# Attention before two expert layers: key-feature sums moved to GpSimd, key exponents read from the projection bank, one maximum for q and k

## The chip, the cores and the metric

The kernel runs on one core of one Trainium2 chip. The metric is the device time of the whole program in microseconds; the times shown are medians over several runs. The profiled execution is a run of its own, with its own time.

## The reference, cut to what matters

```python
def phi(x):                                   # q, k: (4, 8, 576, 64); w_phi: (64, 128)
    proj = np.einsum('bhsd,df->bhsf', x, w_phi)
    proj = proj - np.max(np.abs(proj), axis=-1, keepdims=True)
    return np.concatenate([np.exp(proj), np.exp(-proj)], axis=-1)
q_p, k_p = phi(q), phi(k)
kv = np.einsum('bhsf,bhsd->bhfd', k_p, v)
z = np.sum(k_p, axis=2)
num = np.einsum('bhsf,bhfd->bhsd', q_p, kv)
den = np.einsum('bhsf,bhf->bhs', q_p, z)[..., None] + 1e-06
attn = num / den                              # -> x, (2304, 512)
```

After it come a dense layer (512 to 2048 to 512 with a relu6 gate) and a routed layer with 8 experts. Neither is touched.

## The kernel before, in words

**Tiling.** The 32 heads go in 16 pairs (u = 0 to 15). Each pair has 9 tiles of 128 rows: four for each head, and a tail tile with the last 64 rows of both heads. A tile's 128 features are doubled by the two signs s of the exponent. The tiles are worked in three groups, `GROUPS = [(8, 1), (0, 4), (4, 4)]`: group 0 is the tail tile, groups 1 and 2 have four tiles each (the first two tiles of each head, then the last two).

**One pair, by engine.** TensorE projects a group of q and k into two PSUM banks, one for each, with no second copy (`projections`, L593). VectorE (`differences`, L1080) takes the largest absolute value of each row of k, subtracts it into `dif` in SBUF, and does the same for q. ScalarE makes the key features `pk` from `dif` (`k_features`, L904, two instructions a group). TensorE transposes the q differences (`dif_transposes`, L612) and ScalarE turns these into query features `pq` (`q_features`, L894). TensorE sums keys times values over the tiles (`kv_sums`, L624, bank KVB) and the key features alone (`z_sums`, L639, bank ZB, products with ones, each tile in its own strip of 32 rows). ScalarE copies both to SBUF (`copy_kvt`, L914). TensorE transposes the first (`kv_transposes`, L653) and multiplies the second by `z_pick`, which adds the strips and spreads them over 64 columns (`z_transposes`, L658). ScalarE copies the result (`copy_kv`, L920). TensorE forms numerators and denominators together (`numerators`, L667, `numerator_tails`, L677), and VectorE divides (`pair_out`, L1118) into `x_sb`.

**Order.** Every engine has a program written out by hand. Steps of pair u+1 are put between those of pair u; each engine works strictly in its order, and only semaphores join them. TensorE's order is `both` at L685, ScalarE's L951, VectorE's L1169. `pair_loop` (L310) runs pairs 0 and 1, a loop over pairs 2 to 7, `middle`, and pairs 8 to 14 with `phase` set; the last pair has a program of its own. GpSimd makes constants at the start; in this stage it then only takes two maxima over the partitions (L497, L499).

**Beside it.** The weights of the dense layer arrive in pieces of 128x1024 (SyncE, `load_pieces`). In pairs 0 to 7 VectorE searches each piece for its maximum (`piece_max_of`, L1129). Then come the maximum over the partitions and five small steps for the scale (`weight_scales`, L1160). In pairs 8 to 15 ScalarE writes the high part of each piece (`piece_hi_of`, L926) and VectorE the low part (`piece_lo_of`, L1136). VectorE also keeps the maximum of v (`v_max`, L1121), whose scale is made in pair 14 (`x_scales`, L1199). In the last pair x is scaled (`x_hi` L933, `x_lo` L1208) and transposed (`x_transpose`, L576) for the dense layer.

Of the kernel before, what the change touches and what calls it, by code (L numbers as in the profile page):

```python
# [34 lines left out]
MT = 4  # L35
# [31 lines left out]
def moe_program(nc, qkt_in, v, w_phi, w_in, w_out, w_gate, w_ogate, w1, w2, out, rows, split):  # L67
# [8 lines left out]
    with ctx:  # L76
# [29 lines left out]
        kvt_sb = part(2 * 2 * F).rearrange("p (z s f) -> p z s f", z=2, s=2)  # L106
        kv_sb = part(4 * 2 * DH).rearrange("p (s z h d) -> p s z h d", s=2, z=2, h=2)
        den = part(2 * PT).rearrange("p (a t) -> p a t", a=2)
        mx = part(2 * PT).rearrange("p (w t) -> p w t", w=2)
        v_sb = part(2 * (PT + 1) * DH).rearrange("p (a t d) -> p a t d", a=2, t=PT + 1)  # L110
        tail_ones = part(2 * 32).rearrange("p (h c) -> p h c", h=2)
        z_pick = part(P)
        dif = part(2 * 2 * PT * F).rearrange("p (a w t f) -> p a w t f", a=2, w=2, t=PT)
        assert used[0] <= 3 * UW
        qkt = part(2 * PT * P).rearrange("p (a n) -> p a n", a=2)
# [93 lines left out]
        max_ready = sem("max_ready")  # L209
        dif_transposed = sem("dif_transposed")  # L210
# [3 lines left out]
        z_summed = sem("z_summed")  # L214
# [73 lines left out]
        PROJ, TB, KVB, ZB, NB = (0, 1), (2, 3), 4, 5, 6  # L288
# [160 lines left out]
        def _(pool):  # L449
# [5 lines left out]
            last_row, last_token = pool.alloc_register("last_row"), pool.alloc_register("last_token")  # L455
            pool.reg_mov(last_row, DUMMY - 1)
            pool.reg_mov(last_token, N - 1)
# [14 lines left out]
            step(nc.gpsimd.memset(tail_ones[:], 0.0))  # L472
            step(nc.gpsimd.memset(tail_ones[0:DH, 0, :], 1.0))
            step(nc.gpsimd.memset(tail_ones[DH:P, 1, :], 1.0))
            step(nc.gpsimd.memset(z_pick[:], 0.0))
            for j in range(4):
                step(nc.gpsimd.memset(z_pick[32 * j:32 * j + 1, DH * (j // 2):DH * (j // 2) + DH], 1.0))
# [18 lines left out]
            pool.wait_ge(max_in, 1)  # L496
            nc.gpsimd.partition_all_reduce(s_max[:, 0:3], s_red[:, 0:3], P, RMAX).then_inc(max_out, 1)  # L497
            pool.wait_ge(max_in, 2)
            nc.gpsimd.partition_all_reduce(s_max[:, 3:4], s_red[:, 3:4], P, RMAX).then_inc(max_out, 1)  # L499
# [72 lines left out]
        def _(pe):  # L572
# [20 lines left out]
            def projections(u, a, g):  # L593
# [6 lines left out]
                if g > 0:  # L600
                    pe.wait_ge(dif_ready, u * 6 + 2 * g)
                elif not isinstance(u, int) or u > 0:
                    pe.wait_ge(dif_ready, u * 6)
# [8 lines left out]
            def dif_transposes(u, a, g):  # L612

                t0, n = GROUPS[g]
                pe.wait_ge(dif_ready, u * 6 + (2 * g + 2))
# [4 lines left out]
                for t in range(n):  # L620
                    last = nc.tensor.transpose(ps[:, TB[g % 2], t * P:(t + 1) * P], dif[:, a, 0, t0 + t, :], ident[:])
# [16 lines left out]

            def z_sums(u):  # L639

                if not isinstance(u, int) or u > 0:
                    pe.wait_ge(tails_ready, u)
                for t in (0, 1, MT):
                    for hh in range(2):
                        for j in range(2 if t < MT else 1):
                            lhs = ones[:, 0:32] if t < MT else tail_ones[:, hh, :]
                            row = DH * hh + 32 * j
                            last = nc.tensor.matmul(ps[row:row + 32, ZB, 0:2 * F], lhs,  # L648
                                                    pk[:, at(hh, t + 2 * j), :, :].rearrange("p s f -> p (s f)"),
                                                    start=t == 0, stop=t == (MT, 1)[j])  # L650
                last.then_inc(z_summed, 1)

            def kv_transposes(u):  # L653
                pe.wait_ge(kvt_ready, u * 2 + 1)
                for s in range(2):
                    nc.tensor.transpose(ps[:, KVB, 2 * s * P:2 * s * P + P], kvt_sb[:, 0, s, :], ident[:])
# [844 lines left out]
```

## Time and profile before

| | |
|---|---|
| median of 3 runs | 963.38 us (962.7 to 967.49) |
| profiled execution, its own time | 964.04 us |
| its span | 962.5 us, 20311 instructions |
| TensorE products | 869.5 us busy (90%) |
| TensorE weight loads | 574.2 us (60%) |
| VectorE | 580.6 us (60%) |
| ScalarE | 388.8 us (40%) |
| GpSimd | 74.9 us (8%), 120 instructions |
| mean granted TensorE clock | 0.959 |

The span runs from the first to the last instruction; the execution's time is slightly longer. Busy shares are averages over all stages: the attention stage is the first quarter. A group of instructions carries the line of the code that issues it, the tiles it writes and reads ("arena" holds all tiles of this stage but the raw inputs to it), their shapes, and the count. A product in f32 shows as two records. The idle time in brackets is that of the engine just before the row, with what ended it.

### The profile page before, as it was taken

The numbers are of one execution on the slowest core, as the hardware profiler recorded it, in microseconds if no ns is written. First come the engines' busy times: TensorE is split into PE (matmuls) and PEld (weight loads), VectorE is DVE, ScalarE is ACT, GpSimd is POOL, SyncE is SP. The second block draws the span as 40 slices with busy tenths as digits, with TensorE's granted clock in tenths as the row PEclk, the third lists the DMA queues.
The fourth block names the chain that finished last, engine by engine and source line by source line (L and its number), as shares of the span: only waits on it lengthen the run. The fifth ranks groups of instructions, "written<-read, shape, count | busy, mean of one in ns | idle before, by whom it ended". The sixth has DMA issues, their size and how long they took to land.

```text
span 962.5 us, 20311 instructions
## 1 busy us (share of the span) xinstructions
PE 869.5 (90%) x7480; PEld 574.2 (60%) x7481; DVE 580.6 (60%) x1202; ACT 388.8 (40%) x666; POOL 74.9 (8%) x120
## 2 busy tenths in 40 slices
PE   5999999998899999997999999992499999999990
PEld 3777777777455555553555555552377777777770
DVE  3778788875795987985987987545131322222223
ACT  2445456656456565664656665522010100011011
POOL 1000000000000001001001001011011111111111
PEclk9999999999999999998999999995599999999995
DMA  6243344331565366465266452554317342664110
GB/s 191 92 161 113 132 160 161 128 123 36 192 235 202 143 234 223 162 230 216 97 226 224 156 206 121 201 182 150 103 46 299 137 162 98 228 251 176 44 34 13
DMA packets 44062, 151.36 MB, mean 157 GB/s; under 512 B 7710, under 2 KB 12062, under 8 KB 37856
## 3 DMA queue, kind: packets, MB, share of 16 engines
q1 hardware_dynamic: 38320, 134.14, 39.2%
q0 software_dynamic: 5520, 16.31, 4.9%
q8 instruction: 41, 0.67, 0.3%
q14 instruction: 21, 0.17, 0.1%
q10 hardware_dynamic: 160, 0.07, 0.0%
HBM read 104.72 MB, written 47.21 MB: 158 GB/s over the span
## 4 chain that ended last, share of the span: by engine, by line
PE 57%; PEld 14%; DVE 10%; issue 8%; DMA 4%; PEldq 3%; ACT 2%; SPq 1%; DVEq 0%; POOL 0%; POOLq 0%; ACTq 0%
PE ps L743 19%; PE ps L732 17%; PEld ps L834 10%; PE ps L607 4%; PE ps L634 4%; PE ps L673 3%; PEld ps L846 3%; DVE arena L1087 3%; PE ps L834 2%; PE ps L648 2%; DVE arena L1094 2%; PE ps L846 2%; DMA arena<-split 1%; DVE u_mx L1253 1%; PE ps L661 1%
## 5 line engine op out<-in xcount | busy, mean ns | idle before, releaser
L732 PE MATMUL ps<-arena,w_in_sb 128*128 128x384 f16 x1152 | 203.5, 329 | 6.0 <-issue 6.0
L743 PE MATMUL ps<-w_out_sb,arena 128*128 128x512 f16 x576 | 172.3, 381 | 9.1 <-DVE stage L1341 9.1
L732 PEld LDWEIGHTS ps<-arena,w_in_sb 128*128 128x128 f16 x1152 | 111.4, 99 | 81.7 <-issue 9.2
L1067 ACT ACTIVATE w_in_sb<-ps 128x512 f16<-128x512 f32 x50 | 29.5, 597 | 257.0 <-PE ps L834 241.3
L834 PEld LDWEIGHTS ps<-w_in_sb,arena 128*128 128x128 f16 x2112 | 124.0, 100 | 9.8 <-issue 5.0
L834 PE MATMUL ps<-w_in_sb,arena 128*128 128x128 f16 x2112 | 125.9, 223 | 4.3 <-DMA arena<-split 2.4
L846 PE MATMUL ps<-arena,w_in_sb 128*128 128x512 f16 x528 | 117.5, 379 | 0.0
L743 PE MATMUL ps<-w_out_sb,stage 128*128 128x512 f16 x288 | 109.7, 381 | 0.0
L1442 DVE SCALAR_TENSOR_TENSOR w_in_sb<-ps,w_in_sb 128x512 f16<-128x512 f32 x50 | 34.3, 691 | 113.7 <-ACT w_in_sb L1067 113.7
L743 PEld LDWEIGHTS ps<-w_out_sb,arena 128*128 128x128 f16 x576 | 55.9, 98 | 68.9 <-issue 11.7
L1033 ACT ACTIVATE arena<-relu 128x384 f16<-128x384 f32 x96 | 50.2, 523 | 106.6 <-DVE relu L1336 106.6
L1336 DVE SCALAR_TENSOR_TENSOR relu<-relu,ps 128x384 f32<-128x384 f32 x96 | 53.0, 552 | 64.8 <-ACT relu L1027 64.2
L846 PEld LDWEIGHTS ps<-arena,w_in_sb 128*128 128x128 f16 x528 | 50.8, 98 | 57.1
L1027 ACT ACTIVATE relu<-ps,three,s_h 128x384 f32<-128x384 f32 x96 | 63.8, 665 | 51.2 <-PE ps L732 48.8
L1280 DVE SCALAR_TENSOR_TENSOR arena<-arena,u_up 128x1024 f16<-128x1024 f32 x64 | 79.2, 1278 | 0.0
L1253 DVE TENSOR_REDUCE u_mx<-arena 128x1 f32<-128x1024 f32 x64 | 74.8, 1211 | 3.9 <-DMA arena<-in_moe_w 3.9
L1087 DVE TENSOR_REDUCE arena<-ps 128x4 f32<-128x512 f32 (+1 forms) x96 | 52.9, 551 | 39.2 <-PE ps L607 39.1
L1018 ACT ACTIVATE arena<-arena,u_up 128x1024 f16<-128x1024 f32 x64 | 69.8, 1137 | 2.9 <-DVE u_up L1272 2.4
L673 PE MATMUL ps<-arena 128*128 128x128 f32 x512 | 66.4, 284 | 3.6 <-ACT arena L924 3.6
L1452 DVE TENSOR_SCALAR w_in_sb<-ps,stage 128x512 f32<-128x512 f32 x25 | 18.7, 750 | 78.5 <-PE ps L846 78.5
L673 PEld LDWEIGHTS ps<-arena 128*128 128x128 f32 x512 | 60.4, 194 | 9.2 <-ACT arena L924 7.3
L911 ACT ACTIVATE arena<-arena 128x512 f32<-128x512 f32 (+1 forms) x96 | 45.1, 522 | 45.3 <-DVE arena L1094 45.3
(175 smaller groups left out, 927.5 us busy)
## 6 DMA issues: line engine op xcount, KB each, us to landing
arena<-in_moe_w SPq DMA_DIRECT2D x16, 2048.0 KB, 13.1
split<-arena SPq DMA_DIRECT2D x16, 2048.0 KB, 7.4
arena<-split SPq DMA_DIRECT2D x32, 1024.0 KB, 5.8
arena<-in_qkt SPq DMA_DIRECT2D x15, 576.0 KB, 6.2
stage<-in_moe_w_in SPq DMA_DIRECT2D x16, 512.0 KB, 4.3
stage<-in_moe_w_out SPq DMA_DIRECT2D x16, 512.0 KB, 5.4
w_in_sb<-rows POOLq DMA_DIRECT2D x25, 257.0 KB, 3.0
arena<-in_v SPq DMA_DIRECT2D x32, 128.0 KB, 4.5
```

The source lines that it names most:

```text
L673: last = nc.tensor.matmul(ps[:, NB + hh, t * 2 * DH:(t + 1) * 2 * DH], pq[:, s, c:c + P], kv_of(s, hh), start=s == 0, stop=s == 1)
L732: last = nc.tensor.matmul(ps[:, HB[f % GB], 0:BN], w_in_sb[:, lw, c, f * P:(f + 1) * P], xt[:, a, c, lx, :], start=c == 0 and lw + lx == 0 ...
L743: last = nc.tensor.matmul(ps[:, YB + r, :], g_sb[lg_][:, f % GB, r * P:(r + 1) * P], w_out_sb[:, lw, f, :], start=f == 0 and lg_ + lw == 0 ...
L834: last = nc.tensor.matmul(ps[:, 2 + 2 * a + f // 4, f % 4 * P:(f % 4 + 1) * P], w1_sb[b][:, lw, c, f * P:(f + 1) * P], xgt[:, a, lx, c, :] ...
L846: last = nc.tensor.matmul(ps[:, 6 + a, :], hg[:, a, lh, f, :], w2_sb[b][:, lw, f, :], start=f == 0 and lh + lw == 0, stop=f == EFC - 1 and ...
L1018: nc.scalar.activation(split_sb[:, 0, q_ * Q:(q_ + 1) * Q], raw[b][:, q_ * Q:(q_ + 1) * Q], ACT.Copy, scale=u_up[:, b:b + 1]).then_inc(u_h ...
L1027: nc.scalar.activation(relu3[:, f % GB, :], ps[:, HB[f % GB], 0:BN], ACT.Relu, bias=three[:, 0:1], scale=s_h[:, 0:1]).then_inc(relu3_ready, 1)
L1033: nc.scalar.mul(g_sb[0][:, f % GB, :], relu3[:, f % GB, :], CG / 6.0).then_inc(g_hi, 1)
L1087: nc.vector.tensor_reduce(mx[:, w, t0:t0 + n], src, AX.X, ALU.max, apply_absolute_value=True).then_inc(max_ready, 1)
L1253: nc.vector.tensor_reduce(u_mx[:, q_:q_ + 1], raw[b][:, q_ * Q:(q_ + 1) * Q], AX.X, ALU.max, apply_absolute_value=True).then_inc(u_searche ...
L1280: nc.vector.scalar_tensor_tensor(out=split_sb[:, 1, cols], in0=raw[b][:, cols], scalar=u_up[:, b:b + 1], in1=split_sb[:, 0, cols], op0=ALU ...
L1336: nc.vector.scalar_tensor_tensor(out=relu3[:, f % GB, :], in0=relu3[:, f % GB, :], scalar=6.0, in1=ps[:, HB[f % GB], 0:BN], op0=ALU.min, o ...
```

## The change

The key features are made straight from the projection bank in PSUM: for each tile and sign one exponent over 128x128, with the row maximum as bias (negated by a small new VectorE instruction into `k_neg` for the plain sign). The key half of `dif` and its subtraction are gone. One maximum is taken over the q and k banks together. The sums of the key features over the tiles are additions on GpSimd into `pk_sum` (SBUF), and TensorE multiplies these by 64 columns of ones straight into the place of the spread sums; `z_sums` of before, its copy, `tail_ones`, `z_pick` and `z_transposes` are gone. The high parts of the weight pieces are written by GpSimd, not ScalarE. The two maxima over the partitions stand in GpSimd's new program between its additions. TensorE's order in a pair changes: the key-value sums now come before the projections of group 0, and the transposes of group 2 before the key-value transposes. The projections also wait for `pk_ready`.

```diff
@@ gpsimd
+            def sums(u, n, out, x, y):
+                nc.gpsimd.tensor_tensor(out, x, y, ALU.add).then_inc(sum_step, 1)
+                pool.wait_ge(sum_step, u * 4 + n)
+            def sums_first(u):
+                pool.wait_ge(pk_ready, u * 3 + 2)
+                if not isinstance(u, int) or u > 0:
+                    pool.wait_ge(kv_transposed, u)
+                sums(u, 1, pk_sum[:], pk[:, 0:4:2], pk[:, 1:4:2])
+                for hh in range(2):
+                    rows_ = slice(DH * hh, DH * hh + TAIL)
+                    sums(u, 2 + hh, pk_sum[rows_, hh], pk_sum[rows_, hh], pk[rows_, 2 * MT])
+            def sums_second(u):
+                pool.wait_ge(pk_ready, u * 3 + 3)
+                sums(u, 4, pk_sum[:], pk_sum[:], pk[:, 4:8:2])
+                nc.gpsimd.tensor_tensor(pk_sum[:], pk_sum[:], pk[:, 5:8:2], ALU.add).then_inc(pk_summed, 1)
+            def piece_hi_of(u, a):
+                pool.wait_ge(w_scale, 1)
+                pool.wait_ge(stage_loaded[a], (u - a) * 16 + 32)
+                for w, dst in ((0, w_in_flat), (1, w_out_flat)):
+                    nc.gpsimd.tensor_scalar(dst[:, 0, bass.ds((u - PAIRS // 2) * Q, Q)], stage[:, a, w, :], s_up[:, w:w + 1], None,
+                                            ALU.mult).then_inc(piece_hi, 1)
+            def both(u, a, phase):
+                sums_second(u)
+                if isinstance(u, int) and u == PAIRS - 2:
+                    pool.wait_ge(max_in, 2)
+                    nc.gpsimd.partition_all_reduce(s_max[:, 3:4], s_red[:, 3:4], P, RMAX).then_inc(max_out, 1)
+                if phase:
+                    piece_hi_of(u, a)
+                sums_first(u + 1)
...
+            sums_first(0)
+            both(0, 0, 0)
+            both(1, 1, 0)
+            with pool.Fori(1, PAIRS // 4) as i:
+                both(i * 2, 0, 0)
+                both(i * 2 + 1, 1, 0)
+            weights_max()
+            for u in range(PAIRS // 2, PAIRS - 1):
+                both(u, u % 2, 1)
+            last_pair()
@@ tensor, projections
-                    pe.wait_ge(dif_ready, u * 6 + 2 * g)
+                    pe.wait_ge(dif_ready, u * 3 + g)
+                    pe.wait_ge(pk_ready, u * 3 + g)
@@ tensor, new z_sums
             def z_sums(u):
+                pe.wait_ge(pk_summed, u + 1)
+                for s in range(2):
                     for hh in range(2):
+                        c = (2 * s + 1) * P + DH * hh
+                        last = nc.tensor.matmul(ps[:, KVB, c:c + DH], pk_sum[:, hh, s, :], ones[:, 0:DH], start=True, stop=True)
@@ tensor, both
                 dif_transposes(u, a, 1)
+                kv_sums(u, a)
                 if more:
                     projections(u + 1, 1 - a, 0)
-                kv_sums(u, a)
-                z_sums(u)
+                dif_transposes(u, a, 2)
                 kv_transposes(u)
+                z_sums(u)
                 if more:
                     projections(u + 1, 1 - a, 1)
                 else:
...
-                z_transposes(u)
-                dif_transposes(u, a, 2)
@@ scalar, k_features
-                act.wait_ge(dif_ready, u * 6 + (2 * g + 1))
+                act.wait_ge(neg_ready, u * 3 + (g + 1))
                 if g == 0 and (not isinstance(u, int) or u > 0):
                     act.wait_ge(kv_summed, u)
-                    act.wait_ge(z_summed, u)
-                for s in range(2):
-                    last = nc.scalar.activation(pk[:, t0:t0 + n, s, :], dif[:, a, 1, t0:t0 + n, :], ACT.Exp, scale=1.0 - 2.0 * s)
+                    act.wait_ge(pk_summed, u)
+                for t in range(n):
+                    for s in range(2):
+                        bias = (k_neg, mx[:, 1])[s]
+                        last = nc.scalar.activation(pk[:, t0 + t, s, :], ps[:, PROJ[1], t * F:(t + 1) * F], ACT.Exp,
+                                                    bias=bias[:, t0 + t:t0 + t + 1], scale=1.0 - 2.0 * s)
@@ vector, differences
+                dve.wait_ge(projected, u * 6 + (2 * g + 2))
+                src = ps[:, PROJ[0]:PROJ[0] + 2, 0:n * F].rearrange("p w (t f) -> p w t f", t=n)
+                nc.vector.tensor_reduce(mx[:, :, t0:t0 + n], src, AX.X, ALU.max, apply_absolute_value=True).then_inc(max_ready, 1)
+                dve.wait_ge(max_ready, u * 3 + (g + 1))
+                nc.vector.tensor_scalar(k_neg[:, t0:t0 + n], mx[:, 1, t0:t0 + n], -1.0, None, ALU.mult).then_inc(neg_ready, 1)
...
+                nc.vector.tensor_tensor(dif[:, a, t0:t0 + n, :], src[:, 0],
+                                        mx[:, 0, t0:t0 + n, None].to_broadcast([P, n, F]), ALU.subtract).then_inc(dif_ready, 1)
```

## Rows read from the trace of the kernel before

**Rows 1.** Busy time by stretch: PE, PEld, DVE, ACT, POOL; clock; DMA.

```profile
60.00:100.00 40.00, 38.42 (x389) 29.59 (x390) 31.91 (x66) 17.95 (x45) 0.00 (x0) 1.00 0.44 145
```

**Rows 2.** Timeline of TensorE over one pair: start, duration, instruction.

```profile
87.39 0.49 PE L607 MATMUL ps<-wphi_sb,arena 64*128 64x128 f32 x4 [0.30 <-DVE arena L1094]
...
90.12 1.07 PE L648 MATMUL ps<-arena,ones 128*32 128x256 f32 x16
...
91.55 0.44 PE L656 MATMUL ps<-ident,arena 128*128 128x128 f32 x2
91.92 1.16 PE L607 MATMUL ps<-wphi_sb,arena 64*128 64x128 f32 x16
...
93.56 0.60 PE L621 MATMUL ps<-ident,arena 128*128 128x128 f32 x4
94.40 2.05 PE L673 MATMUL ps<-arena 128*128 128x128 f32 x16 [0.24 <-ACT arena L924]
...
96.97 1.16 PE L607 MATMUL ps<-wphi_sb,arena 64*128 64x128 f32 x16
98.06 2.05 PE L673 MATMUL ps<-arena 128*128 128x128 f32 x16
...
100.95 0.49 PE L607 MATMUL ps<-wphi_sb,arena 64*128 64x128 f32 x4 [0.30 <-DVE arena L1094]
```

**Rows 3.** Timeline of TensorE's weight loads in the routing step.

```profile
361.98 0.30 PEld L778 LDWEIGHTS ps<-onehot,ones 128*128 128x128 f32 x2
```

**Rows 4.** Timeline of VectorE in the same pair.

```profile
98.16 0.69 DVE L1087 TENSOR_REDUCE arena<-ps 128x4 f32<-128x512 f32 x1 [1.18 <-PE ps L607]
...
100.89 0.15 DVE L1103 TENSOR_SCALAR arena<-ps 128x1 f32<-128x1 f32 x1
```

**Rows 5.** Timeline of VectorE and GpSimd at the maximum of the weights.

```profile
131.21 1.21 DVE L1131 TENSOR_REDUCE w_mx<-stage 128x1024 f32 x1
...
132.99 0.39 POOL L497 PARTITION_ALL_REDUCE s_max<-s_red  x1 [125.45 <-DVE s_red L1164]
```

**Rows 6.** Groups by shape on ScalarE: count, busy us, mean ns, idle before.

```profile
L911 ACT ACTIVATE arena<-arena 128x512 f32<-128x512 f32 x64 | 36.9, 630 | 42.6 <-DVE arena L1094 42.6
L900 ACT ACTIVATE arena<-ps 128x512 f32<-128x512 f32 x64 | 34.7, 600 | 0.3 <-PE ps L621 0.3
...
L1004 ACT ACTIVATE yrow<-stage,y_up 128x512 f16<-128x512 f32 x18 | 11.6, 707 | 1.8 <-DVE y_up L1236 1.8
...
L900 ACT ACTIVATE arena<-ps 128x128 f32<-128x128 f32 x32 | 6.8, 262 | 0.0
```

**Rows 7.** Timeline of ScalarE: four query exponents in a row.

```profile
100.66 1.40 ACT L900 ACTIVATE arena<-ps 128x128 f32<-128x128 f32 x4
```

**Rows 8.** Groups by shape on GpSimd.

```profile
L528 POOL MEMSET stage<- 128x513 f32 x1 | 0.6, 555 | 0.0
...
L488 POOL CAST ident<-ident 128x128 f16<-128x128 f32 x1 | 0.3, 289 | 0.1
```

**Rows 9.** Timeline of TensorE after the maximum of the weights.

```profile
138.29 1.16 PE L607 MATMUL ps<-wphi_sb,arena 64*128 64x128 f32 x16 [0.57 <-DVE arena L1094]
```

**Rows 10.** Timeline of VectorE in pair 14, around the maximum of v.

```profile
214.41 0.81 DVE L1126 TENSOR_REDUCE v_mx<-arena 128x1 f32<-128x640 f32 x1
...
217.33 0.68 DVE L1087 TENSOR_REDUCE arena<-ps 128x4 f32<-128x512 f32 x1
```

**Rows 11.** Timeline of TensorE from the last projections to the last numerators.

```profile
220.12 1.16 PE L607 MATMUL ps<-wphi_sb,arena 64*128 64x128 f32 x16 [0.31 <-DVE arena L1094]
...
230.01 0.83 PE L590 MATMUL ps<-ident,yrow 128*128 128x128 f16 x12 [2.10 <-DVE yrow L1211]
...
232.41 2.89 PE L673 MATMUL ps<-arena 128*128 128x128 f32 x16
```

**Rows 12.** Groups by shape on VectorE: the low part of a weight piece.

```profile
L1139 DVE SCALAR_TENSOR_TENSOR w_in_sb<-stage,s_up,w_in_sb 128x1024 f32 x6 | 7.7, 1277 | 0.0
```

More of the change, by code:

```diff
@@ L105, in moe_program @@
         pq = part(2 * PT * P).rearrange("p (s n) -> p s n", s=2)
-        kvt_sb = part(2 * 2 * F).rearrange("p (z s f) -> p z s f", z=2, s=2)
+        kvt_sb = part(2 * F).rearrange("p (s f) -> p s f", s=2)
+        pk_sum = part(2 * 2 * F).rearrange("p (h s f) -> p h s f", h=2, s=2)
         kv_sb = part(4 * 2 * DH).rearrange("p (s z h d) -> p s z h d", s=2, z=2, h=2)
@@ L620, in dif_transposes @@
                 for t in range(n):
[L621 removed]
+                    last = nc.tensor.transpose(ps[:, TB[g % 2], t * P:(t + 1) * P], dif[:, a, t0 + t, :], ident[:])
                 last.then_inc(dif_transposed, 1)
@@ L637, in kv_sums, with kv_transposes @@
                 last.then_inc(kv_summed, 1)
+            def kv_transposes(u):
+                pe.wait_ge(kvt_ready, u + 1)
+                for s in range(2):
+                    nc.tensor.transpose(ps[:, KVB, 2 * s * P:2 * s * P + P], kvt_sb[:, s, :], ident[:])
             def z_sums(u):
-                if not isinstance(u, int) or u > 0:
-                    pe.wait_ge(tails_ready, u)
-                for t in (0, 1, MT):
+                pe.wait_ge(pk_summed, u + 1)
+                for s in range(2):
                     for hh in range(2):
[L645 to L654, printed above, removed]
-                for s in range(2):
-                    nc.tensor.transpose(ps[:, KVB, 2 * s * P:2 * s * P + P], kvt_sb[:, 0, s, :], ident[:])
-            def z_transposes(u):
-                pe.wait_ge(kvt_ready, u * 2 + 2)
-                for s in range(2):
-                    last = nc.tensor.matmul(ps[:, KVB, (2 * s + 1) * P:(2 * s + 2) * P], kvt_sb[:, 1, s, :], z_pick[:], start=True, stop=True)
+                        c = (2 * s + 1) * P + DH * hh
+                        last = nc.tensor.matmul(ps[:, KVB, c:c + DH], pk_sum[:, hh, s, :], ones[:, 0:DH], start=True, stop=True)
                 last.then_inc(kv_transposed, 1)
@@ L981, in last_pair @@
                     copy_xt(0, 0, c, X0[c])
-                for w in range(2):
-                    piece_hi_of(u, a, w)
                 nc.scalar.activation(wg_sb[:, 0], wg_raw[:], ACT.Copy, scale=s_up[:, 2:3]).then_inc(wg_hi, 1)
@@ L1079, in _, with differences @@
         def _(dve):
[L1080 removed]
+            def differences(u, a, g):
                 t0, n = GROUPS[g]
[L1083 to L1096 removed]
+                dve.wait_ge(projected, u * 6 + (2 * g + 2))
[3 more added lines that the diff above has]
+                nc.vector.tensor_scalar(k_neg[:, t0:t0 + n], mx[:, 1, t0:t0 + n], -1.0, None, ALU.mult).then_inc(neg_ready, 1)
+                if g == 0 and (not isinstance(u, int) or u > 1):
+                    dve.wait_ge(dif_transposed, u * 3 - 3)
+                nc.vector.tensor_tensor(dif[:, a, t0:t0 + n, :], src[:, 0],
+                                        mx[:, 0, t0:t0 + n, None].to_broadcast([P, n, F]), ALU.subtract).then_inc(dif_ready, 1)
             def normalise(u, a, b, j):
```

102 lines of the change are left out of this document (38 added, 64 removed).

## The prediction

> **What bounds the kernel now.** I read the page first (engine shares, the 40 slices), then busy time by stretch, then the timeline of one steady pair engine by engine, the waits, and the two places where GpSimd takes a maximum. The attention stage, which alone is changed, ends near 240 us. From 60 to 100 us TensorE is busy 38.42 of 40 us, VectorE 31.91, ScalarE 17.95, GpSimd not at all [rows 1]. One pair repeats every 13.56 us (87.39 to 100.95) [rows 2]. I take it apart by start times: projections of group 0 with the key-value sums 2.73, key sums (L648) 1.43, their transposes (L656) 0.37, projections of group 1 1.09, spreading transposes (L661) 0.55 (what is left before 93.56), query transposes of group 2 0.60 and a wait of 0.24, numerators and tails 2.57, projections of group 2 1.09, other numerators and transposes 2.59, a wait of 0.30 for the difference of q. The sum is 13.56. So TensorE sets the pace, with 0.54 of waiting; what it no longer has to do is a gain only until a chain through another engine sets in.
>
> **TensorE's edits.** The key sums (1.43) and spreading (0.55) go. In their place stand 4 products, 8 records of 128x128 f32 weights against 64 columns. No such shape is in the trace. A record of the numerators, same weights and 128 columns, takes 2.05/16 = 0.13, nearer 0.12 without the last one's tail; one of the projections, half the rows, 1.09/16 = 0.07 [rows 2]; two loads of such weights before 24 columns take 0.30, so at most 0.15 each [rows 3]. Loads, not columns, set it, so I take 0.11, just under the numerators: 0.88 in all (0.55 to 1.2). 1.10 us of work per pair is saved, and moving the projections of group 0 behind the sums removes the 0.30 wait. Nothing else on TensorE changes in amount.
>
> **The chain that takes over.** Projection banks are single. Until now VectorE read them and freed them; now ScalarE reads the key bank for its exponents, and TensorE waits for pk_ready before it writes the next group. I walk it from the start of a group of 4: TensorE to VectorE 1.19 (96.97 to 98.16), about 0.06 more as q is projected last [rows 2, 4]; one maximum over 1024 values 1.21, as the maximum of the same size in the weight search [rows 5]; the sign flip, a 128-row by few-column instruction, 0.15 with 0.05 ahead of it [rows 4]; a hand-over of 0.04; then 8 exponents of 128x128 where two of 128x512 stood. From PSUM one takes 0.262 alone, the 512 form 0.600 [rows 6]; four of them in a row (two of each) took 1.40 against 1.72 added, so neighbours overlap by 0.11 [rows 7]. A per-partition operand costs 0.08 (0.707 against 0.630, both from SBUF) to 0.107 (against 0.600) [rows 6]. I take 0.09: 0.25 a piece, 7 x 0.25 + 0.35 = 2.10. With 0.04 to TensorE the chain is 4.84. Bounds: 4.1 if the operand costs nothing in a row of them (7 x 0.15 + 0.26 = 1.3), 5.2 if it costs twice as much and the overlap halves.
> Between group 1 and group 2 TensorE has 1.09 + 2.57 = 3.66 to do. So it now waits 1.2 us there in each pair, which eats the saving.
>
> **The pair after.** Count from the start of group 2's projections. Group 2 1.09; numerators and transposes 2.59, to 3.68; sums of tiles 0, 1 and tail (six tenths of 2.31) to 5.07, while pk_ready of group 2 comes at 4.84, so no stall; sums and group 0 end at 6.41; transposes of group 2 7.01; the key-value transposes 7.38 (their copy on ScalarE ends by 6.7: exponents to 4.8, four of q to 6.1, and a copy of 256 columns, under 0.6). Now TensorE needs GpSimd's sum. GpSimd starts its two additions at 4.86. The first half (one addition of 512 and two of 256 on 64 rows) lies in the 4.8 us before, with room. Then products to 8.26, group 1, and 4.84 later the next group 2: 13.10. ScalarE's copy of kv (0.6) and query exponents end 1.8 after group 1 starts, before their 2.7; VectorE's search (1.21) and v maximum end at 9.4, its next work is due at 9.5. Gain: 0.46 a pair.
>
> **The additions.** GpSimd has never added here. Bounds per addition of 512: 0.56, one write of 513 columns; 2.3, two inputs each at four times the 0.289 of a 128-column cast [rows 8]. I take four casts, 1.16, since a cast already reads and writes: done at 4.86 + 2 x 1.16 + 0.1 = 7.28, against 7.38. There is just no stall. The sum's arrival also frees ScalarE, whose exponents of the next pair's group 0 now wait for it with the copy of kv queued behind them: 7.28 + 0.6 = 7.9, before group 1 at 8.26, so nobody waits for that. The Trainium skill ("GPSIMD Engine Reference", Performance versus the Vector engine) gives 4497 ns for a two-input f32 addition over 2048 columns and about 2.6 cycles an element; that is an estimate of 1.1 to 1.2 for 512, on the value taken, and no row here shows one. Above 1.21 each further 0.1 costs 0.2 a pair: a stall of 2.2 a pair at the upper bound.
> Moving the scaling of weight pieces to GpSimd frees ScalarE of work (two pieces of 1024 columns a pair, from u = 8) that was already off the path; on GpSimd they fill 7.3 to at most 12 (eight casts each, 2.3), before its next sum at 13.1. The small constants that fall away at the start were nobody's wait, and SyncE's loads follow the same semaphores in the same order, now slightly earlier: both at nothing.
>
> **Two places where GpSimd's order costs.** (a) The maximum over the weights now stands in GpSimd's stream before the second half of pair 8. VectorE hands it over only after the differences of group 0 of pair 9 and the last piece's search. The search starts at 7.35 of that pair; from there to GpSimd's reduction is 1.78 (131.21 to 132.99), the reduction 0.39 [rows 5], then two additions, 2.4: sum at 11.9 instead of 7.3. TensorE loses 4.5 once, where it lost 0.57 before [rows 9]. (b) The maximum over v in pair 14: VectorE's v maximum starts at 8.5, and from its start to the next differences 2.92 pass (214.41 to 217.33) [rows 10], so these begin at 11.4 instead of 9.5: 1.9 on the chain that now has no slack, against 0.31 before [rows 11]. Together 5.5 more than before.
> **The last pair.** The input transposes wait for the scaled x as before: 9.89 after the last projections [rows 11]. After them stood spreading and query transposes until the numerators, 232.41 - 230.01 = 2.40; now only the transposes themselves, 0.83 less the tail of the last, about 0.7 as an estimate: 1.7 less.
>
> **Sum**, against the profiled execution (span 962.5, its time 964.04, 0.66 over the median of 963.38): 15 pairs x 0.46 = 6.9 less, 1.7 less, 5.5 more: 3.1 less, 960.9, which is 960.3 against the median. Some 0.5% (4.8 us) is what can be told from no change, so faster means under 958.6, slower over 968.2.
>
> **Rivals.** *GpSimd's additions become the bound* (slower). It decides from 1.31 us an addition: each 0.1 over 1.21 costs 0.2 x 15 plus 0.2 in pair 8, so 3.2. At 1.5 the result is 960.3 + 9.3 = 969.6. For it: two inputs have to be read, and the upper bound lies far off; against it: four casts hold their fixed time four times, an addition once.
> *VectorE and GpSimd hold each other up.* From pair 9 VectorE's low part (two inputs in SBUF, 1.28 [rows 12]) and GpSimd's high part start within 0.1 us of each other, at 7.3. If one must stand still while the other runs, VectorE loses up to a high part, 1.2 to 2.3 by the cast, less its 0.1 of slack: the next maximum comes 1.5 later in pairs 9 to 13, and x's low part in the last pair by 1: 8 more, 968.5. For it: both read the same stage tile in that moment; against it: which starts first is open, and if VectorE does, nothing is lost. The Trainium skill ("SBUF — State Buffer", Who interferes with whom) states this as an exclusive lock when VectorE has two SBUF inputs and GpSimd reads SBUF; no row here shows a GpSimd read beside such an instruction, so the trace neither agrees nor differs; by the rule the time is this rival's if GpSimd starts first, and the forecast's if VectorE does.
> *The exponents are cheaper in a row* (the operand's 0.09 hides behind the one before): the chain falls to 4.1 and with half of that to 4.5; 0.4 to 0.7 a pair more, 949 to 955, say 954. For it: the 0.262 overlap nearly half; against it: 0.707 against 0.630 is plain.
> *The change brings nothing*: the kept time is lost to small stalls on VectorE, whose margins at 9.4 and 4.84 are 0.1 and 0.2: 963.5.
>
> **Chances.** Forecast 0.40, additions the bound 0.20, cheap exponents 0.20, lock 0.14, nothing 0.06. Forecast alone: 957 to 964. The range goes from 952 to 971, which leaves out the cheapest exponents and additions over 1.55. Faster: 0.20 + 0.12 of the forecast = 0.32; same: 0.27 + 0.06 + 0.07 of the two slower rivals = 0.40; slower 0.28.
>
> **What would show it.** Starts of group 2's projections 13.1 apart with a TensorE idle of 1.2 just before, released by ScalarE: the chain is right. Idle before the 4 new products: the additions are too long, and their mean says by how much. Exponents about 0.35 each, 0.25 apart. Pair 8 some 4.5 longer. VectorE idle or late before the group 1 maximum only from pair 9: the lock. Wrong if the wait before group 2 is under 0.8, or if pairs of the first and second half differ by over 0.3.

## The result and the profile after

| | before | after |
|---|---|---|
| median | 963.04 us (960.31 to 967.49) | 998.35 us (996.15 to 999.17) |
| ratio | | 1.0359, interval 1.0315 to 1.0402 |
| profiled span | 962.5 us | 996.1 us |
| TensorE products busy | 869.5 us | 860.6 us |
| ScalarE busy | 388.8 us | 401.8 us |
| GpSimd busy | 74.9 us | 209.7 us |

The changed kernel is 3.6% slower. I had forecast 960.3 us and had given slower a chance of 0.28; even my range ended at 971. Hardly any of the loss is in the steady pair. TensorE's projections of group 2 are a mark that both traces have. In pair 1 they start at 27.25 us (before 29.07), in pair 8 at 124.09 (before 124.08): what the seven pairs between lose, 1.8 us, the start had won. Nearly all of the 33.6 us of span are lost in three places, and at each of them GpSimd changes between additions and the maximum over the partitions.

GpSimd's timeline after, around the maximum of the weights (start us, us, engine, line, operation, shapes, count, and in brackets the idle time before it with what ended it):

```profile
124.03 2.86 POOL L492 TENSOR_TENSOR arena<-arena 128x512 f32<-128x512 f32 x3 [6.04 <-ACT arena L951]
133.20 0.39 POOL L528 PARTITION_ALL_REDUCE s_max<-s_red  x1 [6.31 <-DVE s_red L1186]
143.94 1.25 POOL L492 TENSOR_TENSOR arena<-arena 128x512 f32<-128x512 f32 x1 [10.35 <-issue]
145.26 1.26 POOL L507 TENSOR_TENSOR arena<-arena 128x512 f32<-128x512 f32 x1
```

The reduction takes 0.39 us, as in [rows 5]. The addition behind it has all its data, yet it starts 10.35 us later, and the idle time is put down to "issue", which means that nothing the profile shows ended it. TensorE's timeline after, in the same pair (it answers to [rows 9]):

```profile
131.11 0.38 PE L692 MATMUL ps<-ident,arena 128*128 128x128 f32 x2
146.58 1.97 PE L700 MATMUL ps<-ones,arena 128*128 128x64 f32 x8 [15.09 <-POOL arena L507]
148.48 2.08 PE L657 MATMUL ps<-wphi_sb,arena 64*128 64x128 f32 x16
150.49 2.55 PE L712 MATMUL ps<-arena 128*128 128x128 f32 x16
...
154.58 1.16 PE L657 MATMUL ps<-wphi_sb,arena 64*128 64x128 f32 x16 [0.95 <-ACT arena L951]
```

TensorE stands for 15.09 us where I had allowed 4.5. Behind the stall its records also run slow, 2.08 us for projections that take 1.16 elsewhere; in the busy times by stretch the granted clock of 140 to 180 us is 0.86, with 1.00 in the 40 us of [rows 1], and taken finer it is 0.50 from 146 to 150 us, 0.61 to 152 and 1.00 behind. By their starts these products, projections and numerators take 2.3 us more than in a steady pair. From group 2 of this pair to that of the next are 30.49 us, 16.3 more than before.

The second place is pair 14, the third the first unit of the dense layer. GpSimd's timeline after:

```profile
229.93 1.26 POOL L507 TENSOR_TENSOR arena<-arena 128x512 f32<-128x512 f32 x1
236.99 0.38 POOL L521 PARTITION_ALL_REDUCE s_max<-s_red  x1 [5.80 <-issue]
244.33 2.85 POOL L514 TENSOR_SCALAR w_in_sb<-stage,s_up 128x1024 f16<-128x1024 f32 x1 [6.96 <-issue]
...
290.87 0.38 POOL L552 PARTITION_ALL_REDUCE u_all<-u_red  x1 [26.48 <-issue]
```

TensorE's timeline after, from the last projections on (it answers to [rows 11]):

```profile
242.58 2.08 PE L657 MATMUL ps<-wphi_sb,arena 64*128 64x128 f32 x16 [6.57 <-ACT arena L951]
...
253.52 1.60 PE L684 MATMUL ps<-arena 128*64 128x256 f32 x8 [3.69 <-ACT arena L951]
...
259.00 1.48 PE L638 MATMUL ps<-ident,yrow 128*128 128x128 f16 x12
260.28 2.02 PE L712 MATMUL ps<-arena 128*128 128x128 f32 x8
```

Group 2 of the last pair is 18.99 us behind that of pair 14 (before 14.03, [rows 11]), and from there to the last numerators are 17.70 us (before 12.29). The account against before: the start 1.8 less, seven pairs 1.8 more, pair 8 16.3, pairs 9 to 13 1.2 (69.01 against 67.80), pair 14 5.0, the last pair 5.4; together 27.9 at the last numerators. The first reduction of the dense layer, at 254.98 before, comes 35.9 later, the third 34.0 later, the end 33.6.

The steady pair after, in TensorE's timeline (it answers to [rows 2]):

```profile
96.44 1.16 PE L657 MATMUL ps<-wphi_sb,arena 64*128 64x128 f32 x16 [1.28 <-ACT arena L951]
...
103.45 0.38 PE L692 MATMUL ps<-ident,arena 128*128 128x128 f32 x2
104.22 1.10 PE L700 MATMUL ps<-ones,arena 128*128 128x64 f32 x8 [0.39 <-POOL arena L507]
105.26 1.16 PE L657 MATMUL ps<-wphi_sb,arena 64*128 64x128 f32 x16
...
110.27 1.16 PE L657 MATMUL ps<-wphi_sb,arena 64*128 64x128 f32 x16 [1.28 <-ACT arena L951]
```

The period is 13.83 us, with the wait of 1.28 on ScalarE's exponents that I had forecast (1.2), and one of 0.39 on GpSimd that I had not. The other engines in this pair, in the timeline after, show how GpSimd's sum comes to be late:

```profile
98.91 0.36 DVE L1113 TENSOR_SCALAR arena<-arena 128x4 f32<-128x4 f32 x1
...
99.30 2.17 ACT L951 ACTIVATE arena<-ps,arena 128x128 f32<-128x128 f32 x8 [3.00 <-DVE arena L1113]
...
101.55 1.28 POOL L492 TENSOR_TENSOR arena<-arena 128x512 f32<-128x512 f32 x1 [2.31 <-ACT arena L951]
...
102.90 1.26 POOL L507 TENSOR_TENSOR arena<-arena 128x512 f32<-128x512 f32 x1
```

### The profile page after: what moved, and what is told of

Its sections match the earlier page's. It is cut to its first block, busy times and chain, and to the rows that moved or that the text cites. A ratio compares the mean times of both kernels' runs of the same rounds, so it can differ in the third digit from the quotient of the medians.

```text
span 996.1 us, 20022 instructions
## 1 busy us (share of the span) xinstructions
PE 860.6 (86%) x7224; PEld 575.5 (58%) x7225; DVE 561.7 (56%) x1154; ACT 401.8 (40%) x826; POOL 209.7 (21%) x208
## 4 chain that ended last, share of the span: by engine, by line
PE 44%; issue 14%; PEld 14%; DVE 8%; POOL 6%; ACT 5%; DMA 3%; PEldq 3%; SPq 1%; POOLq 0%; ACTq 0%; DVEq 0%
PE ps L781 17%; PE ps L770 15%; PEld ps L872 10%; ACT arena L951 4%; POOL arena L492 4%; PEld ps L884 3%; PE ps L657 3%; DVE arena L1111 2%; POOL arena L507 2%; PE ps L872 2%; PE ps L700 2%; PE ps L884 2%; DMA arena<-split 1%; DVE u_mx L1275 1%; DVE y_mx L1253 1%
## 5 line engine op out<-in xcount | busy, mean ns | idle before, releaser
L951 ACT ACTIVATE arena<-ps,arena 128x128 f32<-128x128 f32 x288 | 79.5, 380 | 115.6 <-DVE arena L1113 81.8
L1111 DVE TENSOR_REDUCE arena<-ps 128x8 f32<-128x1024 f32 (+1 forms) x48 | 46.0, 958 | 79.7 <-PE ps L657 79.7
L492 POOL TENSOR_TENSOR arena<-arena 128x512 f32<-128x512 f32 (+1 forms) x64 | 64.6, 1009 | 101.2 <-ACT arena L951 88.4
L657 PE MATMUL ps<-wphi_sb,arena 64*128 64x128 f32 x576 | 49.0, 306 | 34.3 <-ACT arena L951 29.8
L552 POOL PARTITION_ALL_REDUCE u_all<-u_red x16 | 7.7, 483 | 326.1 <-DVE u_red L1279 299.6
```

The lines of the kernel that those rows point to most:

```text
L492: nc.gpsimd.tensor_tensor(out, x, y, ALU.add).then_inc(sum_step, 1)
L657: done = nc.tensor.matmul(ps[:, PROJ[w], t * F:(t + 1) * F], qkt[DH * w:DH * w + DH, a, c:c + P], wphi_sb[DH * w:DH * w + DH, :], start=Tr ...
L951: last = nc.scalar.activation(pk[:, t0 + t, s, :], ps[:, PROJ[1], t * F:(t + 1) * F], ACT.Exp, bias=bias[:, t0 + t:t0 + t + 1], scale=1.0 ...
L1111: nc.vector.tensor_reduce(mx[:, :, t0:t0 + n], src, AX.X, ALU.max, apply_absolute_value=True).then_inc(max_ready, 1)
```

## The experiments

Two theories. *Theory 1*: on GpSimd a change between the additions (or the scaling) and the reduction costs 6 to 10 us each way, and this is the whole loss. *Theory 2*, on the steady pair: the sums on GpSimd are a gain, and the exponents from the projection bank give it back, since their chain ends later than TensorE's work.

**Constants in place of the reductions.**

```diff
-                nc.gpsimd.partition_all_reduce(s_max[:, 0:3], s_red[:, 0:3], P, RMAX).then_inc(max_out, 1)
+                nc.gpsimd.tensor_copy(s_max[:, 0:3], s_known[:, 0:3]).then_inc(max_out, 1)
...                                                          # and the same for 3:4
```

> The changed kernel, with its two maxima over the partitions in this stage left out: GpSimd copies constants of the right exponent in their place, at the same point of its order. Theory 1: what costs most is not the reduction (0.39) but the time around it, in which GpSimd issues nothing that the trace shows: 10.35 us after the first reduction, 5.8 before the second and 6.96 after it. A plain copy has no such time. Then TensorE's wait in pair 8 falls from 15.1 to about 4.7, VectorE's wait for the v scale from 4.2 to under 0.5, and its wait of 6.4 for the high part in pair 14 goes: some 20 to 23 us less, 976 to 979. Rival: the waits come from the order of GpSimd's program, as predicted, and from how full it is; then the copy saves only the two reductions, about 1 us, and the time stays at 997.

Measured: 979.01 us, ratio 1.0172 (1.0147 to 1.0197). GpSimd's timeline of this kernel:

```profile
133.39 0.18 POOL L532 COPY s_max<-s_known 128x3 f32<-128x3 f32 x1 [6.25 <-DVE s_red L1190]
133.54 1.26 POOL L496 TENSOR_TENSOR arena<-arena 128x512 f32<-128x512 f32 x1
```

With a copy in the place of the reduction the next addition starts at once, TensorE's stall falls from 15.09 to 4.45 us (I had forecast 4.5 for a reduction without any such gap), and 19 us are gone. So the gaps are there and cost that much; that the wait for the maximum itself made the whole stall is out. But they are not the whole loss, as theory 1 had it. TensorE's timeline of this kernel:

```profile
136.20 1.97 PE L704 MATMUL ps<-ones,arena 128*128 128x64 f32 x8 [4.45 <-POOL arena L511]
138.09 2.08 PE L661 MATMUL ps<-wphi_sb,arena 64*128 64x128 f32 x16
```

The stall is now the one that I forecast, and yet the records behind it are slow again: the granted clock is 0.50 from 136 to 142 us, and by their starts the same steps take 2.9 us more than in a steady pair. My prediction had no term for that. Of the 16.8 us left over the kernel before, 8.8 stand at group 2 of the last pair (228.92 against 220.12, 6.2 of them from pair 8), and the first unit's reduction, at 271.05 with 26.38 of "issue" ahead of it, is 16.1 late: the third place is still there.

**The reduction called once ahead of the dense layer.**

```diff
 def last_pair():
     ...
+    nc.gpsimd.partition_all_reduce(warm[:, 1:2], warm[:, 0:1], P, RMAX)   # result unused
```

> The changed kernel, with one more maximum over the partitions, of a scratch column, at the end of GpSimd's attention program. Theory 1: the first use of the reduction after ordinary instructions costs about 6 us; put where GpSimd is idle it is hidden, and the first unit maximum of the dense layer comes about 6 us earlier after its request, which gives back the 4.8 us that the changed kernel loses behind the attention stage: about 993.5. Rival: that loss comes from something else (the stage loads, the clock), and nothing changes: 998.

Measured: 994.52 us, ratio 1.0328 (1.0305 to 1.0351), 3.8 us under the changed kernel. The first unit's reduction now comes at 283.15 and is ended by VectorE's data, not by "issue". The third place is a change of the same kind. The reduction called early pays the gap itself, 6.03 us of "issue", where nothing waits for it. The interval overlaps that of the changed kernel (1.0315 to 1.0402), and the span is 2.3 us shorter (993.8 against 996.1), so the gain is some 2 to 4 us.

**A row of operations on an idle GpSimd, in the kernel before.**

```diff
+for one in (copy_, add_, add_, reduce_, reduce_, copy_, copy_, reduce_, add_, add_, reduce_, copy_, reduce_):
+    one()
```

> The kernel before, with a row of GpSimd instructions added where it is idle: copy, add, add (128x512), reduction, reduction, copy, copy, reduction, add, add, reduction, copy, reduction, each waiting for the one before. Theory 1: every step from an ordinary instruction to the reduction has a gap of about 6 us, every step back one of 7 to 10 us, and steps between equals have about 0.1. Rival: the gap belongs to the first use alone, or to waits on other engines: then only the first reduction has a gap. An addition takes 1.2 to 1.3. The time of the kernel stays at that of before either way, as all of it lies before the weight maximum at 133 us.

Measured, in GpSimd's timeline of this kernel:

```profile
8.78 0.19 POOL L504 COPY cnt<-cnt 128x1 f32<-128x1 f32 x1
9.05 2.61 POOL L507 TENSOR_TENSOR relu<-relu 128x512 f32<-128x512 f32 x2
18.48 0.83 POOL L501 PARTITION_ALL_REDUCE cnt<-cnt  x2 [6.83 <-issue]
19.38 0.43 POOL L504 COPY cnt<-cnt 128x1 f32<-128x1 f32 x2
19.90 0.35 POOL L501 PARTITION_ALL_REDUCE cnt<-cnt  x1
27.00 2.61 POOL L507 TENSOR_TENSOR relu<-relu 128x512 f32<-128x512 f32 x2 [6.75 <-issue]
35.59 0.38 POOL L501 PARTITION_ALL_REDUCE cnt<-cnt  x1 [5.98 <-issue]
```

The price stands by itself here: 6.83 and 5.98 us into the reduction, 6.75 back to the addition, each time anew. Between reduction and copy there is none, which I had expected to be a change too: that part was a miss. It also explains why the copy in the first experiment was free beside the additions. The price lies between additions and reduction, not between any two kinds of work. The time, 963.18 us in a single run, within the range of the kernel before (961.11 to 964.92), shows no cost of any of it where GpSimd has nothing else to do.

**The high parts back on ScalarE**, otherwise the changed kernel.

> The changed kernel, with the high parts of the weight pieces back on ScalarE. Theory 1: GpSimd has room for them in a steady pair (the pairs of the second half are no longer than those of the first, 13.77 against 13.83), so only pair 14, where they stand behind the reload, gains: 3 to 6 us less, 992 to 995. Rival (GpSimd is overfull, and it and VectorE hold each other up): every pair from 9 on gets shorter by 0.5 or more and pair 14 as well: 10 us or more less, under 988.

Measured: 992.52 us, ratio 1.0313 (1.0289 to 1.0337). The timeline after shows what GpSimd's high parts and VectorE's low parts do to each other:

```profile
162.01 1.44 DVE L1161 SCALAR_TENSOR_TENSOR w_out_sb<-stage,s_up,w_out_sb 128x1024 f32 x1
...
162.34 3.81 POOL L514 TENSOR_SCALAR w_in_sb<-stage,s_up 128x1024 f16<-128x1024 f32 x1
...
166.14 2.84 POOL L514 TENSOR_SCALAR w_out_sb<-stage,s_up 128x1024 f16<-128x1024 f32 x1
...
166.63 1.70 DVE L1161 SCALAR_TENSOR_TENSOR w_in_sb<-stage,s_up,w_in_sb 128x1024 f32 x1
```

Where VectorE is first (162.01), GpSimd's part takes 3.81 us instead of 2.84: 0.97 more, nearly the 1.11 that VectorE's instruction still had to run. Where GpSimd is first (166.14), its part keeps its 2.84, and VectorE's takes 1.70 instead of 1.28 [rows 12], but ends at 168.33, before GpSimd's. (The 1.44 of the first one is not this: with the parts on ScalarE it takes 1.43 as well.) So they hold each other up, VectorE the less. On the path this costs 0.06 us at most: from group 1 to group 2 pass 5.07 us in the second half and 5.01 in the first. A pair of the second half takes 13.77 us with the parts on GpSimd and 13.90 with them on ScalarE. What the move back wins, it wins in the last two pairs, where VectorE's low part no longer waits 6.39 us for a GpSimd that is on its way back from the reduction (input transposes at 255.37 instead of 259.00).

**Each half of the change alone.** First the sums on GpSimd with TensorE's new order, the key exponents and the maxima of q and k as before, the high parts on ScalarE and constants for the maxima over partitions; then the exponents from the projection bank and the one maximum, with the key sums as before and the key-value sums moved up in TensorE's order. In both, ScalarE writes the two high parts of a pair behind the exponents of group 1.

> The kernel with known constants for the two maxima (979.0), and the key half undone: VectorE subtracts the maxima of k into dif again, one maximum for each of q and k, ScalarE takes 2 exponents of 128x512 a group and writes the high parts behind them; the sums stay on GpSimd. Theory 2: in a steady pair the saving on TensorE is eaten by the chain from one projection bank through ScalarE's 8 exponents to the next (5.0 us against 3.7 us of other work); the additions by themselves cost nothing. Then with the key half undone the chain is 3.97 (as in the kernel before), the wait before group 2 falls from 1.3 to 0.3 or 0.5, the additions start 1.1 earlier and their wait goes: a pair takes 12.4 to 12.6, and 15 pairs at 1.2 less and a smaller stall in pair 8 give 957 to 961. Rival: GpSimd's additions are the cost, and VectorE's subtraction that comes back makes it the bound: the pair stays at 13.5 or more, the time at 974 or more.

> The kernel before, with the key half of the change alone: exponents from the projection bank with the maximum as bias, one maximum for q and k, the key-value sums ahead of the projections of group 0; key sums and their spreading stay on TensorE, both reductions over the partitions on GpSimd as before, high parts on ScalarE behind the exponents. Theory 2: TensorE here has the spreading (0.55) and the transposes (0.6) between group 1 and group 2 as well, 5.0 in all, as long as the chain; so the exponents cost nothing, both waits of before (0.54) go, and a pair takes 13.1 to 13.2: 955 to 958. Rival: the exponents make every pair longer whatever stands beside them, by the wait of 1.3 seen in the changed kernel: 970 or more.

Measured: the sums alone 956.09 us, ratio 0.9944 (0.9926 to 0.9961), faster than the kernel before. TensorE's timeline of this kernel:

```profile
85.63 1.16 PE L648 MATMUL ps<-wphi_sb,arena 64*128 64x128 f32 x16 [0.60 <-DVE arena L1120]
...
92.47 0.38 PE L683 MATMUL ps<-ident,arena 128*128 128x128 f32 x2
92.69 1.00 PE L691 MATMUL ps<-ones,arena 128*128 128x64 f32 x8
...
97.95 1.16 PE L648 MATMUL ps<-wphi_sb,arena 64*128 64x128 f32 x16 [0.59 <-DVE arena L1120]
```

A pair of the first half takes 12.32 us, 1.24 less than before and 1.51 less than after. GpSimd's sum is there in time (the key features come earlier), and the wait before group 2 is 0.60 instead of 1.28. In the second half a pair takes 12.94 to 13.08, so the gain is only some 0.6: VectorE's low part waits 1.16 us for ScalarE's high part with the differences of group 2 queued behind, the sum is late by as much, and TensorE waits 0.44 for it. Pair 8, even with constants, takes 19.93 us (before 14.21).

The exponents alone: 986.51 us, ratio 1.0258 (1.0233 to 1.0283). I had expected 955 to 958; the rival, 970 or more, came true, and theory 2 had this half too cheap. TensorE's timeline of this kernel:

```profile
95.47 1.16 PE L612 MATMUL ps<-wphi_sb,arena 64*128 64x128 f32 x16 [0.71 <-ACT arena L918]
...
97.95 2.05 PE L678 MATMUL ps<-arena 128*128 128x128 f32 x16 [0.24 <-ACT arena L932]
...
101.09 1.16 PE L612 MATMUL ps<-wphi_sb,arena 64*128 64x128 f32 x16 [0.50 <-ACT arena L918]
```

The pair takes 14.54 us in the first half. Its work is 13.09, as I had said; the waits of 0.71, 0.24 and 0.50 are the rest. Since ScalarE now frees the projection bank, whatever stands before the exponents in ScalarE's order holds TensorE's next projections: the exponents of the tail tile wait for the copy of the key sums, which TensorE has only just made, and those of group 1 for the copy of kv and two query exponents. In the second half a pair takes 15.68: TensorE waits another 0.92 for the exponents of group 2, whose maximum is queued on VectorE behind a low part that waits for ScalarE's high parts (1.23 us each). How much of this is owed to where the high parts stand, and not to the exponents, was not tested apart. Theory 2 holds in its direction only: its reason, that the chain is longer than TensorE's work, does not explain waits of 1.21 where the two are equal; ScalarE's order does. In the first half the exponents cost a pair 1 us by themselves (14.54 against 13.56), and GpSimd's sums alone win 1.24. Together they give 0.27 more, not 0.26 less: with late exponents GpSimd's sum is late too, and TensorE waits for it (0.39), and before group 2 it waits 1.28 us instead of 0.60.

**A version with the true maxima.** The maxima over the partitions go through DRAM, a store of 128 rows and a load spread to all partitions, so that GpSimd never leaves its additions in this stage; the reduction is called early once.

```diff
+sp.dma_start(maxima[k], s_red[:, cols]) ...
+sp.dma_start(relu3[:, 0, 0:n], maxima[k] ... .to_broadcast([P, n])) ...
+... nc.vector.tensor_reduce(s_max[:, 0:3], relu3[:, 0, 0:3 * P] ..., AX.X, ALU.max) ...
```

> The sums on GpSimd without the key half, and with the true maxima: VectorE's maxima of each partition go to DRAM and back to all partitions by SyncE's DMAs, VectorE takes the last maximum, and picks it up one step later in pairs 8 and 14; one reduction of a constant at the end of GpSimd's attention program calls for its code early. By theories 1 and 2: the steady pair of 12.4 to 12.6, no wait around a reduction, and the 4.8 behind the stage given back: 949 to 954, faster than before. Rival: the round trip through DRAM (two DMAs behind the piece loads) is late and costs what it saves: 960 or more.

Measured: 957.92 us, ratio 0.9959 (0.9944 to 0.9974). Faster than before, but 4 us over what I had expected: VectorE waited 3.80 us for the load of the weight maximum, with the differences of group 2 queued behind (pair 8 took 18.5), and TensorE 7.92 before the input transposes. The second store was slow, as its row among the DMA issues of this kernel shows (tiles, engine, count, KB, us to landing):

```profile
maxima<-s_red SPq DMA_DIRECT2D x1, 1.5 KB, 2.2
maxima<-s_red SPq DMA_DIRECT2D x1, 0.5 KB, 8.0
```

**Three follow-ups.** The sums alone with the early call; then two ways to place the exchange.

> The kernel with the key sums on GpSimd alone and constants for the four maxima over partitions, and one more reduction, whose result nobody reads, called at the end of GpSimd's attention work. Theory 1 (each change between additions and the reduction costs GpSimd 6 to 10 us): the first unit of the dense layer waits some 4 to 5 us less, as VectorE's 6.3 us wait there showed; 951 to 953 us, against 956.1 without that call. Rival (the 26 us before that first reduction is not code but the wait for the unit, so an early call does nothing here): 955.5 to 957 us.

Measured: 955.12 us (949.84 to 956.46), ratio 0.9911 (0.989 to 0.9932); span 952.9 against 956.3 without the call. The first unit's reduction moves from 252.01 to 244.96 us, as theory 1 says. What it is worth in time is less clear: 955.12 lies between the two forecasts, the spans say 3.4 us and the medians 1.0, and the two intervals of the ratio touch (0.989 to 0.9932, 0.9926 to 0.9961).

> The key sums on GpSimd alone with the true maxima exchanged through DRAM, and everything that uses them moved later: the weight scales after the division of pair 8, the pieces' low parts one pair behind, the x scale after the division of pair 14, and the second store wider (12 bytes a partition instead of 4, as the first, which took 2.2 us where the second took 8.0). Theory 2 (what is left in the kernel with GpSimd sums is waiting on VectorE and ScalarE behind these exchanges): pair 8 falls from 18.5 us to 14 to 16, the wait before the input transposes from 7.9 us to 2 to 5: 949 to 953 us against 957.9. If the width of the store is not what made it slow: the wait before the input transposes stays above 4.5 us and the time is 952 to 955. Rival (the two places are covered by the dense layer's start anyway): 956 to 958 us.

Measured: 957.53 us, ratio 0.9944 (0.9924 to 0.9964): the rival's time. The wide store did land in 2.2 us, and the wait before the transposes fell from 7.92 to 1.78 us, yet they started at 223.95, later than the 222.57 of the version before: TensorE's wait had only moved, 6.99 us of it into the key-value sums. Pair 8 took 17.75, not 14 to 16. With the low parts a pair later the stage tiles came free later, the last weight piece was loaded later, and ScalarE stood in front of it, the exponents of group 2 queued behind. ScalarE's timeline of this kernel:

```profile
214.80 1.15 ACT L971 ACTIVATE w_in_sb<-stage,s_up 128x1024 f16<-128x1024 f32 x1 [9.04 <-DMA stage<-in_moe_w_out]
```

So what one edit won was given back by the other; the next version puts this to the test.

> The kernel with the key sums on GpSimd alone and the true maxima exchanged through DRAM, with the low parts and the weight scales where they were there (pair 8 stays at 18.5 us), but the second store 12 bytes a partition wide instead of 4, issued before SyncE's wait for the low parts, and the x scale taken after the division of pair 14 instead of before it. Theory (a store of 4 bytes a partition takes 8.0 us and of 12 bytes 2.2, and nothing behind it is lost when the weight loads keep their place): the second store lands in 2.2 us, the input transposes start 4 to 5 us earlier than at 222.57, 952 to 954.5 us, ratio to the kernel before near 0.991. Rival (the gain at the end of the attention stage is covered by the dense layer's start, where the first unit's reduction is waited for anyway): transposes earlier, time 956 to 958.

Measured: 949.76 us (944.98 to 951.3), ratio 0.9883 (0.9853 to 0.9913), better than expected and the lowest median of all (its interval overlaps that of the sums alone with the early call). TensorE's timeline and the DMA issues of this kernel:

```profile
217.65 1.44 PE L636 MATMUL ps<-ident,yrow 128*128 128x128 f16 x12 [3.24 <-DVE yrow L1256]
...
maxima<-s_red SPq DMA_DIRECT2D x2, 1.5 KB, 2.2
```

The transposes start 4.9 us earlier than at 222.57, and both stores take 2.2 us. The store was issued at 203.06 us, against 203.35 there, so the earlier issue gained nothing; how the 4.9 divide between the wider store (5.8 us sooner) and the division put ahead of the x scale was not separated. This kernel keeps the half of the change that wins, leaves out the half that costs, and takes GpSimd's reduction out of the additions' way.

## Why the prediction was wrong, step by step

- **The step that failed** is "two places where GpSimd's order costs". I priced each reduction at its own 0.39 us [rows 5] and added only the wait for its data, 5.5 us for both. The runs showed 6 to 10 us before and behind a reduction that stands between additions, in pair 8, in pair 14 and, a third place that I had not looked at, ahead of the dense layer. Without the reductions 19 of the 35 us are gone. Pair 8 shows it best: I had TensorE lose 4.5 us, and with a copy in the reduction's place it lost 4.45; with the reduction 15.09. A second term I had put at nothing: behind either stall TensorE's granted clock was 0.50, worth 2.3 and 2.9 us. The row that I took the price from was of a GpSimd that had been idle for 125.45 us, as the bracket of [rows 5] says: whatever came before the reduction was hidden in it.
- The Trainium skill ("GPSIMD Engine Reference", 2.1 Instruction dispatch) says that the first call to freshly loaded code costs about 6 us (5.95) and shows no instruction in the profile. The gaps into the reduction agree (5.80, 5.98, 6.83); that it comes again at each change, and as much on the way back to additions or scaling (6.75, 6.96, 10.35), is what these runs add.
- **The steady pair**: forecast 13.10, measured 13.83. The chain to the exponents 4.84, measured 5.01 (91.43 to 96.44): the maximum (1.23) and the eight exponents (2.17 in a row, mean 0.38 each) were nearly right, and the rest is the hand-over to TensorE, 0.15 instead of 0.04. The eight products 0.88, measured 1.04 (90.39 to 91.43). The additions 1.16 each, measured 1.27 and 0.08 between them; and they started at 5.11 of the pair instead of 4.86, mostly because the sign flip of group 2 took 0.36 instead of 0.15. So the sum came at 7.73 instead of 7.28 and TensorE waited 0.39. These three errors, 0.17, 0.16 and 0.39, are the whole difference. Each was inside its bounds; together they turned a gain of 0.46 a pair into a loss of 0.27, about 11 us over 15 pairs. Of the 38 us between 960.3 and 998.35, the other 27 lie in pair 8 (12), pair 14 (3), the last pair (7) and the dense layer (6), with 1 won back at the start. The upper bound of the chain was added wrongly: an operand at twice the price and half the overlap give 5.9 by the prediction's own terms, not 5.2.
- **Rivals.** "GpSimd's additions become the bound" did not come true: they took 1.27 us, under the 1.31 from which I let it decide, and by my own rule (0.2 for each 0.1 over 1.21) they are 0.12 of the wait of 0.39; the later start is the rest. "VectorE and GpSimd hold each other up" happens, but not as a lock that makes VectorE stand still: VectorE started first and lost nothing to the high part, GpSimd lost 0.97, and where GpSimd was first VectorE lost 0.42 and still ended first. TensorE's path felt 0.06 of it a pair. The exclusive lock that the prediction cites is thus borne out in one direction only, that of GpSimd coming second. "The exponents are cheaper in a row" is out.
- **The last pair**: 1.7 less was forecast, 5.4 more came, since VectorE's maximum of group 2, and x behind it, were queued behind a low part that waited 6.39 us for GpSimd's return to the scaling.
- My marks would have told the steady pair right (idle of 1.28 before group 2, released by ScalarE) but pair 8 "some 4.5 longer" was 16.3 longer, and that decided.

That the gap is the loading of code is an inference from its place, its size and its independence of data; the profile shows only that nothing ended it. Why it was 10.35 us in pair 8 (10.32 and 10.33 in the two other kernels with a reduction there) and 6.75 to 7.19 elsewhere stays open, and so does why the sign flip took 0.36 in group 2.

## What to carry to other kernels

Before an engine that takes different kinds of work is given one more kind, look at what surrounds each kind in the trace: a duration read beside a long idle time says nothing of what it costs to get there. On GpSimd a reduction over partitions between additions cost some 6 us on the way in and 7 to 10 on the way back, so a stream of additions has to be kept clear of it, and the reduction called once, early, where the engine idles. When the reader of a PSUM bank changes from one engine to another, everything that stands ahead in the new reader's order is put between the bank and its next writer; take the halves of such a change apart, since one may be a gain and the other a loss.

## What was not expected of the hardware

- GpSimd: 5.56 to 6.83 us (once 7.93) without a visible instruction into the reduction over partitions and 6.75 to 10.35 us back to additions or scaling, at every change; none between the reduction and a copy.
- A store of 128 rows of 4 bytes to DRAM took 8.0 us, one of 12 bytes a row 2.2 us. The wide form was seen five times in three kernels, the narrow one once, so a chance cause of the 8.0 is not excluded.
- A GpSimd scaling of 1024 columns from f32 to f16 took 2.84 us alone, and 3.81 when it started 0.33 us behind a VectorE operation with two SBUF inputs. When it started first it kept its 2.84, and VectorE's operation went from 1.28 to 1.70, or to 2.15 where both started together.
- After a stall of 15.09 us TensorE's records took up to twice their time for some 4 us (1.97 for products that take 1.10 elsewhere), at a granted clock of 0.50, the level of 1.2 GHz; this is within the 16.3 us of pair 8. After a stall of 4.45 us the same records took 1.97 as well, and the clock was 0.50 for 6 us.
